# Fused attention and feed-forward: first batch on other PSUM banks, early first-layer chunks, w_in split by GpSimd, constants in one load

## The reference

```python
# q, k, v: (4, 12, 448, 64), cap = 30, w_in (768, 2048), w_out (2048, 768)
scores = cap * np.tanh(scale * np.matmul(q, k.transpose(0, 1, 3, 2)) / cap)
scores = scores - np.max(scores, axis=-1, keepdims=True)
attn = np.exp(scores)
attn = attn / (np.sum(attn, axis=-1, keepdims=True) + 1e-09)
x = np.matmul(attn, v)            # then (batch * 448, 12 * 64)
r = np.maximum(x @ w_in, 0.0)
y = (s * (r * r) + b) @ w_out
```

## Time and profile before

| what | value |
|---|---|
| median of 3 runs | 653.55 us (652.8 to 655.07) |
| the profiled execution | 654.5 us |
| its span in the profile | 652.7 us |
| mean granted clock of PE | 0.987 |
| PE busy | 632.1 us (97%) |
| DVE, ACT, POOL busy | 345.3, 246.1, 37.0 us |

### The profile page before, as it was taken

How to read it: one execution, slowest core, us unless ns; L and a number is a source line. 1 busy time by engine, 2 the same in 40 slices (tenths; PEclk the granted TensorE clock), 3 DMA queues, 4 the chain that set the end, 5 groups by cost and what they waited for, 6 DMA issues and landing times.

```text
span 652.7 us, 7957 instructions
## 1 busy us (share of the span) xinstructions
PE 632.1 (97%) x3146; PEld 490.6 (75%) x3146; DVE 345.3 (53%) x587; ACT 246.1 (38%) x255; POOL 37.0 (6%) x28
## 2 busy tenths in 40 slices
PE   5989989979999999999999999999999999999998
PEld 3333657656767676767677999999999999999997
DVE  1699999997767667767665433222432131213111
ACT  4788444544444544454541322222321121213110
POOL 0122333420000000000000000000000000000000
PEclk8899989998999999999999999999999999999999
DMA  5344143422222222313111411213152233215002
GB/s 167 116 140 140 57 141 115 158 62 99 87 69 88 82 73 83 100 57 101 40 57 44 159 49 49 68 54 109 50 191 57 57 121 105 57 30 183 1 1 84
DMA packets 32148, 57.14 MB, mean 88 GB/s; under 512 B 3952, under 2 KB 23920, under 8 KB 32112
## 3 DMA queue, kind: packets, MB, share of 16 engines
q1 hardware_dynamic: 31680, 56.64, 26.8%
q10 hardware_dynamic: 432, 0.00, 0.0%
HBM read 40.11 MB, written 16.52 MB: 87 GB/s over the span
## 4 chain that ended last, share of the span: by engine, by line
PE 81%; DVE 13%; ACT 3%; issue 2%; DMA 1%; POOLq 0%; POOL 0%; ACTq 0%; DVEq 0%
PE hid L345 10%; PE hid L347 10%; PE hid L346 10%; PE scores L360 8%; PE scores L361 8%; PE scores L359 8%; PE pv L304 5%; PE scores L270 5%; PE pv L360 4%; PE pv L361 4%; PE pv L359 4%; PE scores L289 2%; DVE w_hi L503 2%; DVE e_sum L522 1%; PE pv L316 1%
## 5 line engine op out<-in xcount | busy, mean ns | idle before, releaser
L345 PE MATMUL hid<-x_hi,w_hi 128*128 128x448 f32 x384 | 144.6, 377 | 6.5 <-POOL w_lo L669 6.5
L347 PE MATMUL hid<-x_hi,w_lo 128*128 128x448 f32 x384 | 142.3, 371 | 0.0
L346 PE MATMUL hid<-x_lo,w_hi 128*128 128x448 f32 x384 | 142.2, 370 | 0.0
L360 PE MATMUL scores<-x_lo,w_hi 128*128 128x448 f32 x256 | 93.5, 365 | 0.0
L359 PE MATMUL scores<-x_hi,w_hi 128*128 128x448 f32 x256 | 93.5, 365 | 0.0
L361 PE MATMUL scores<-x_hi,w_lo 128*128 128x448 f32 x256 | 93.5, 365 | 0.0
L345 PEld LDWEIGHTS hid<-x_hi,w_hi 128*128 128x128 f32 x384 | 73.4, 191 | 24.9 <-issue 19.0
L595 DVE SCALAR_TENSOR_TENSOR x_lo<-e,const,x_hi 128x448 fp32r<-128x448 f32 x48 | 32.1, 683 | 103.8 <-ACT x_hi L447 103.8
L347 PEld LDWEIGHTS hid<-x_hi,w_lo 128*128 128x128 f32 x384 | 73.3, 191 | 6.4
L346 PEld LDWEIGHTS hid<-x_lo,w_hi 128*128 128x128 f32 x384 | 73.5, 191 | 6.0
L433 ACT ACTIVATE e<-e,const 128x1792 f32<-128x1792 f32 (+1 forms) x48 | 77.0, 1604 | 1.6
(11 more groups left out here) (67 smaller groups left out, 666.0 us busy)
## 6 DMA issues: line engine op xcount, KB each, us to landing
qk<-q_k SPq DMA_DIRECT2D x24, 448.0 KB, 3.8
hidden_scratch<-hidden_sb SPq DMA_DIRECT2D x48, 224.0 KB, 1.9
e<-hidden_scratch SPq DMA_DIRECT2D x48, 224.0 KB, 2.6
work<-w_in SPq DMA_DIRECT2D x24, 256.0 KB, 3.5
e<-w_out SPq DMA_DIRECT2D x16, 384.0 KB, 3.0
y_t<-qk SPq DMA_DIRECT2D x24, 224.0 KB, 2.0
v_sb<-v SPq DMA_DIRECT2D x24, 192.0 KB, 2.6
v_tail<-v SPq DMA_DIRECT2D x12, 64.0 KB, 2.3
```

The source lines that it names most:

```text
L345: nc.tensor.matmul(out, w_hi[:, j, w], x_hi[:, batch % 2, c, :], start=c == 0, stop=False)
L346: nc.tensor.matmul(out, w_hi[:, j, w], x_lo[:, batch % 2, c, :], start=False, stop=False)
L347: last = nc.tensor.matmul(out, w_lo[:, j, w], x_hi[:, batch % 2, c, :], start=False, stop=c == CT - 1)
L360: nc.tensor.matmul(y_acc(c), w_hi[:, j, w], ring(x_lo, n), start=False, stop=False)
```

## The change

1. One tensor, banks, of eight PSUM banks: 0 to 3 are scores, 4 and 5 hid, 6 and 7 pv. In the first batch pair p's products lie in pv[p % 2] and its sums in pv[(p + 1) % 2], the bank of the neighbouring pair. The second groups of pairs 1 to 5 are written to hid's banks, and the tails of a quad to banks 2 and 3. Pair 0 has all its groups at once on eight banks, with two tanh for the second.
2. PE's order in the first batch: last_scores(p + 1) stands before values(p), tail_values is done pair by pair, and sums waits for xt of the pair before. EARLY = 12 chunks of the first layer run before the pair loop of the second batch, around pair 6's last scores; the other 84 are 14 per pair.
3. GpSimd makes w_hi and w_lo, six pieces at the start, four more casts, and the rest after the sixth x_done. DVE's casts are gone, and its order in the first batch is add_last, scale_pair, add_first, invert_first.
4. cap, s and b come in one DMA, and half of qk 0 is loaded by ACT's queue. The guard is computed after pair 0's exponentials.
5. From pair 6 on the transposition of e_sum is part of the reduction (apply_transpose).

```diff
-        scores = ctx.enter_context(nc.psum_tensor("scores", [P, G1, BANK], F32))
-
-        pv = ctx.enter_context(nc.psum_tensor("pv", [P, 2, BANK], F32))
-        hid = ctx.enter_context(nc.psum_tensor("hid", [P, 2, BANK], F32))
+        banks = ctx.enter_context(nc.psum_tensor("banks", [P, 8, BANK], F32))
+        scores = banks[:, 0:G1]
+
+        hid = banks[:, G1:G1 + 2]
+
+        pv = banks[:, G1 + 2:G1 + 4]
...
         def pv_out(p):
-            return first_banks(p)[:, 0, 0:S] if p < PAIRS else pv[:, p % 2, 0:S]
+            return pv[:, p % 2, 0:S]
+
+        def sums_out(p):
+
+            return pv[:, (p + 1) % 2, 0:S]
+
+        def products(p):
+
+            return p + 1 if p < PAIRS else PAIRS + (p - PAIRS) // 2 + 1
+
+        def last_group(p):
+
+            return p + 2
+
+        def chunks_of(batch, c):
+
+            if batch == 0:
+                share = (CHUNKS - EARLY) // PAIRS
+                return EARLY + share * c, EARLY + share * (c + 1)
+            return SHARE * c, SHARE * (c + 1)
...
+                of = p - QK_SLOTS
+                if of >= 0:
+                    sp.wait_ge(first_done, of + 1)
+                    sp.wait_ge(last_done, of + 1)
+                    sp.wait_ge(tails_done, of // 2 + 1)
...
-            load_qk(0)
+
+            sp.dma_start(qk[0:D, 0].rearrange("p a n -> p (a n)"), q_k[0, 0, 0:D]).then_inc(qk_in[0], 16)
             load_qk(1)
             load_v(0)
             load_w_in(0)
             load_w_in(1)
+            load_qk(2)
+            load_w_in(2)
+            load_w_in(3)
             load_v(1)
-            load_qk(2)
-            for p in range(PAIRS):
+            load_v(2)
+            load_w_in(4)
+            load_qk(3)
+            load_w_in(5)
+            load_w_in(6)
+            load_v(3)
+            load_w_in(7)
+            load_w_in(8)
+            load_w_in(9)
+            for p in range(2, PAIRS):
+                load_qk(p + 2)
                 load_v(p + 2)
-                load_qk(p + 3)
-                load_w_in(p + 2)
-            load_w_in(PAIRS + 2)
-            load_w_in(PAIRS + 3)
 
             for p in range(PAIRS, ALL):
                 batch, c = divmod(p, PAIRS)
                 if p + 2 < ALL:
+                    load_qk(p + 2)
                     load_v(p + 2)
-                if p + 3 < ALL:
-                    load_qk(p + 3)
                 if batch == 1 and c < 4:
...
             def first_scores(p):
-                i = p % QK_SLOTS
-                pe.wait_ge(qk_in[i], 16 * (p // QK_SLOTS + 1))
-
-                reach(pe, tanh_done, 2 * p)
-                for t in range(FULL - 1):
+                pe.wait_ge(qk_in[p % QK_SLOTS], qk_loads(p))
+
+                reach(pe, first_read, p)
+                if p <= PAIRS:
+                    for head in range(2):
+                        row_scores(p, head, 0, head)
+                    if p % 2 and p > 1:
+                        pe.wait_ge(last_read, last_group(p - 1))
+                    for head in range(2):
+                        last = row_scores(p, head, 1, 2 + head)
+                else:
+                    pe.wait_ge(last_read, last_group(p - 1))
+                    for t in range(FULL - 1):
+                        for head in range(2):
+                            last = row_scores(p, head, t, 2 * t + head)
+                last.then_inc(first_done, 1)
...
+            def last_scores(p, bank):
+                for head in range(2):
+                    last = row_scores(p, head, FULL - 1, bank + head)
+                last.then_inc(last_done, 1)
+
+            def tail_scores(quad, bank):
+
+                pe.wait_ge(qk_in[(2 * quad + 1) % QK_SLOTS], qk_loads(2 * quad + 1))
+                for odd in range(2):
+                    of = (2 * quad + odd) % QK_SLOTS
+                    out_rows = slice(odd * D, (odd + 1) * D)
                     for head in range(2):
                         rows = slice(head * D, (head + 1) * D)
...
+                        last = nc.tensor.matmul(banks[out_rows, bank + head, 0:S], qk[rows, of, 1, FULL * P:],
+                                                qk[rows, of, 0, :], start=True, stop=True)
+                last.then_inc(tails_done, 1)
...
-                pe.wait_ge(exp_done, 2 * (p + 1))
-
+
+                if p == 0:
+                    pe.wait_ge(last_read, last_group(0))
                 reach(pe, x_done, p - 1)
+                reach(pe, sums_read, min(p, PAIRS))
+                pe.wait_ge(exp_done, 2 * p + 1)
                 for t in range(FULL):
+                    if t == FULL - 1:
+                        pe.wait_ge(exp_done, 2 * (p + 1))
...
             def sums(p):
-                out = first_banks(p)
+                out = sums_out(p)
                 pe.wait_ge(e_sum_done, 3 * (p + 1))
-                reach(pe, sums_read, p - 1)
+
+                reach(pe, x_done, p)
                 for head in range(2):
                     rows = slice(head * D, (head + 1) * D)
-                    last = nc.tensor.matmul(out[rows, 1, 0:S], ones[:], e_sum[:, p % 2, head, :], start=True, stop=True)
+                    last = nc.tensor.matmul(out[rows], ones[:], e_sum[:, p % 2, head, :], start=True, stop=True)
...
             first_scores(0)
-            last_scores(0)
+            last_scores(0, G1)
+            tail_scores(0, G1 + 2)
             for p in range(PAIRS):
                 first_scores(p + 1)
+                if p + 1 < PAIRS:
+                    pe.wait_ge(last_read, last_group(p))
+                    last_scores(p + 1, G1)
                 values(p)
-                if p % 2:
-                    tail_values(p // 2)
-                last_scores(p + 1)
+                tail_values(p, 1)
+                if p % 2 and p + 1 < PAIRS:
+                    pe.wait_ge(first_read, p + 2)
+                    tail_scores((p + 1) // 2, 2)
                 sums(p)
+
+
+            for c in range(CT - 1):
+                hidden_chunk(0, c)
+            pe.wait_ge(first_read, PAIRS + 1)
+            tail_scores(PAIRS // 2, 0)
+            last_scores(PAIRS, 2)
+            for c in range(CT - 1):
+                hidden_chunk(0, CT + c)
+            for j in range(2):
+                hidden_chunk(0, CT * j + CT - 1)
...
-                    tail_values(p // 2)
+                    tail_values(p - 1, 2)
                 if p + 1 < ALL:
-                    last_scores(p + 1)
-                for chunk in range(SHARE * c, SHARE * (c + 1)):
+                    pe.wait_ge(first_read, p + 2)
+                    if p % 2:
+                        tail_scores((p + 1) // 2, 0)
+                        last_scores(p + 1, 2)
+                    else:
+                        last_scores(p + 1, 0)
+                for chunk in range(*chunks_of(batch - 1, c)):
...
+                if p == 0:
+                    nc.scalar.activation(e[:, TAIL:TAIL + 2, :], hid[:, :, 0:S], ACT.Tanh, scale=tanh_scale
+                                         ).then_inc(last_read, 1)
+                    nc.scalar.activation(e[:, G1:TAIL, :], pv[:, :, 0:S], ACT.Tanh, scale=tanh_scale
+                                         ).then_inc(last_read, 1)
+                    return
+                if p < PAIRS:
+                    source = banks[:, G1:G1 + 2, 0:S] if p % 2 else banks[:, 2:2 + 4, 0:S]
+                else:
+                    source = banks[:, 0:2, 0:S] if p % 2 else banks[:, 0:4, 0:S]
+                nc.scalar.activation(e[:, group_of(p, 1), :], source, ACT.Tanh, scale=tanh_scale).then_inc(last_read, 1)
...
-            act.dma_start(cap_c, cap.broadcast_to([P, 1])).then_inc(const_in, 16)
-            act.dma_start(s_c, s.broadcast_to([P, 1])).then_inc(const_in, 16)
-            act.dma_start(b_c, b.broadcast_to([P, 1])).then_inc(const_in, 16)
+            act.dma_start(const[:, 0:3], consts.broadcast_to([P, 3])).then_inc(const_in, 16)
+            act.dma_start(qk[D:P, 0].rearrange("p a n -> p (a n)"), q_k[0, 0, D:P]).then_inc(qk_in[0], 16)
             act.wait_ge(const_ready, 1)
-            nc.scalar.activation(const[:, 6:7], abs_cap, ACT.Exp, scale=-1.0).then_inc(guard_done, 1)
-            act.wait_ge(guard_done, 1)
-            nc.scalar.mul(guard_c, const[:, 6:7], GUARD).then_inc(guard_done, 1)
             for p in range(PAIRS + 1):
                 first_tanh(p)
                 exponential(p, 0)
                 last_tanh(p)
                 exponential(p, 1)
...
+            for j in tiles_in(0, EARLY):
+                rectify(j)
...
+                nc.vector.tensor_reduce(parts[:], e_sum[:, p % 2].rearrange("p h (n i) -> p (h n) i", i=BLOCK), AX.X,
+                                        ALU.add, apply_transpose=True).then_inc(parts_done, 1)
...
-            dve.wait_ge(guard_done, 2)
             add_first_e(0)
-            add_last_e(0)
             for p in range(PAIRS):
-                w_in_high(p)
+                add_last_e(p)
+                if p == 0:
```

(60 more changed lines are left out.)

131 lines of the change are left out of this document (55 added, 76 removed).

## The result

| what | before | changed |
|---|---|---|
| median of the runs | 653.53 us (651.22 to 655.07) | 657.64 us (656.9 to 658.46) |
| ratio, 95% interval | | 1.0061 (1.0036 to 1.0086) |
| the profiled execution, its span | 654.5, 652.7 us | 656.9, 654.9 us |
| mean granted clock of PE | 0.987 | 0.990 |
| PE busy | 632.1 us | 632.5 us |

One of six executions of the changed kernel took 1038 us at a mean granted clock of 0.557 and stands apart from all others; it is left out here. The change makes the kernel slower by 0.6%, 4 us, where 16 us less were forecast; the result lies outside the range.

What follows compares the result with a forecast made beforehand. PE's work, waits and lower-clock losses were taken to bound the kernel, with VectorE and ScalarE almost full. Terms 6.0 + 11.3 - 1.3 = 16.0 us off the profiled 654.5; from the median 653.55, forecast 637.5 us, range 632.5 to 645.0.

Steps and rivals of the forecast that it cites:

- the w_lo waits: Hid's matmuls on PE: both waits for w_lo from GpSimd go, with their lower clock, 11.3 us gained.
- Rival 2: Hid's matmuls: one w_lo wait stays or comes anew, 643.5 us; both stay, 648.8 us; chance 0.14.
- rival 3: GpSimd's w_in casts are dear and delay q and k of pair 4: slower, up to 662.3 us; chance 0.03.
- the chance of 0.03 for slower: Whole kernel: slower than before by one mechanism, rival 3's dear GpSimd cast; chance 0.03.
- First batch: PE up to pair 7's scores: 6.0 us gained, from 3.9 to 8.4.
- the change of stages: Where chunks 5 and 11 wait for x of pair 5: 1.3 us charged for one or two gaps.
- The start: Pair 0: first scores kept at 5.55 us, first tanh at 8.65 behind a table load, 0.65 us sooner.
- Landmarks: PE's times in the first batch: pair 2's scores at 19 to 21 us, pair 3's at 29.0, pair 7's at 58.1.
- GpSimd on VectorE's port: From 16 to 27 us, VectorE's two-input instructions each pay up to 1.0 us; first-batch gain 5.6 us instead of 8.4.
- Sum: Whole kernel: 6.0 + 11.3 - 1.3 = 16.0 us off, forecast 637.5 us; chance 0.62.
- the signs named as proving it wrong: PE waits for w_lo, pair 4's q and k land after 32 us, or PE waits over 3 us between 19 and 56.
- the signs of being right: Profile: first tanh near 8.65 us, hid's first matmul near 56, no w_lo wait, clock 1.00 from 60, GpSimd casts under 2.

Runs made afterwards that it cites:

- the kernel with the loads in order: The changed kernel with q and k of pair p + 3 again requested at step p from the second batch on, ahead of the stores: 638.27 us.
- the cut kernel: The kernel with the loads in order, with GpSimd's casts and subtractions of the first ten w_in pieces cut to 32 of 512 columns: 638.45 us.
- the kernel with the guard first: The kernel with the loads in order, with the guard's two ScalarE instructions back before pair 0's first tanh: 637.39 us, repeat 637.38 us.

## Why the prediction was wrong

**The step that failed** is in the part on the w_lo waits: "The next six pieces are loaded after two stores of hidden, from 82". I set the stores of hidden and w_in's loads against each other in SP's queue, but gave the loads of q and k there no deadline. The diff moves them by one step, from pair p + 3 to pair p + 2, and I priced that move at nothing without naming it; the list of the change does not name it either, only the diff has it. A line for it would have read: pair 9 is issued behind the stores of the step, at about 86, lands 4 to 5 us later, and is needed by the tail scores at 85. The premise of the quoted sentence was off too: with the early chunks it is four stores, the last of which has left SP at 86.0, and the pieces of w_in go from 87.03. Rival 2 saw that "SP's queue holds w_in behind stores", but looked at w_in alone, and gave it one wait of 6.0 us; rival 3 looked at q and k of pair 4, ahead of all stores. What measured 13.1 us of waits and 4.6 of clock was in no case of mine, and the chance of 0.03 for slower had nothing to do with it.

**The other steps** can be read from the changed kernel up to 66 us, and from the kernel with the loads in order behind it:

- *First batch*, 6.0 forecast less 1.3 for the change of stages, 4.7 together. In the kernel with the loads in order pair 7's scores start at 66.44, with 7.3 us of early chunks done: 63.67 - 59.1 = 4.5. The sum came right by luck, as two errors cancel. The start gave 1.1 less than forecast (first tanh at 9.74), as I kept 5.55 us for the first scores and PE's warm-up ended at 6.5. The change of stages cost no wait at all: PE has no gap between 56.67 and 66 us, so 1.3 was too much.
- *Landmarks.* Pair 2's scores were laid out for 19.3 to 20.6, and came at 20.98; pair 3's for 29.0, and came at 29.29; pair 5's sums for their end at 56, and ended at 56.7.
- *GpSimd on VectorE's port.* The adds of 1.09 grew to 1.64 and 1.38 us, as forecast in kind. The layout had them cost 2.2 us up to the sums of pair 1 (28.0 instead of 25.8); the cut kernel bears out 1.3 to 1.5, by the two workings above. The cast was 0.61 us in the median (1.49 at most), and not 0.9. The Trainium skill, "GPSIMD Engine Reference", section "Elementwise — side-by-side cycle accounting", gives about one cycle per element for such a loop; at the 1.2 GHz of its example that is 0.44 us for 512 elements, an estimate. The trace has 0.17 us more, so the 0.6 of the prediction holds a fixed part that this figure does not give.
- *The w_lo waits*, 11.3. Of the 16.2 us of span between the kernel before and the kernel with the loads in order, 4.5 are the first batch and 11.7 the rest. With casts back on VectorE, 10.1 of them were lost again. Right in kind and size.
- *Sum.* 637.5 was forecast, and 638.27 was measured once the order of the loads was put back. The 0.8 us between are smaller than the two errors that cancel in the first batch, so the closeness is luck in part.

Of the signs named as proving it wrong none appeared: no wait for w_lo, q and k of pair 4 issued at 24.4, and 1.7 us of waits between 19 and 56 us. The signs guarded the steps I had thought of. Of the signs of being right, "a clock of 1.00 from 60 us on" was the one that failed.

## What to carry to other kernels

When a diff changes an index in a queue's program, write for each moved request two times: when the last thing ahead of it in that queue can end, and when its first reader needs it. A queue that holds both loads and stores gives every load the stores' dependencies, here the inversion of sums on VectorE, two steps away from the store; move loads ahead of stores, or give them another queue. And where a long wait hides a second one, taking away either one alone tells too little: try the order by itself, on both kernels.

## What the runs showed that I had not expected

**The warm-up's length.** The same 50 warm-up passes took 5.35 to 5.60 us in most of the kernels built on the change, 4.82 in two, and 4.48 in the repeat of a kernel that had taken 5.38. From 4 to 5 us the kernel before made 20 passes, and the changed one 13, while the granted clock is given as 1.00 in both. The two executions of the kernel with the guard first differ in the same way:

```profile
4.00:5.00 1.00, 1.00 (x13) 1.00 (x12) 0.20 (x2) 0.41 (x2) 0.00 (x0) 1.00 1.07 283
```

```profile
4.00:5.00 1.00, 1.00 (x20) 1.00 (x19) 0.21 (x2) 0.41 (x2) 0.00 (x0) 1.00 1.06 290
```

When PE comes to full pace at the start differs between two executions of one program by about 1 us, and the row of the granted clock does not show it. The Trainium skill, "TensorE: Matmul & The Clock Gate", in its part on the clock gate, says that the number of slow matmuls at a kernel's start varies from run to run; the two executions agree. What decides it was not tried.

**The split load.** q and k of pair 0 in two halves on two queues landed at about 6.2 us where PE waited for them (0.4 to 0.7 us in four of the kernels), later than the whole load in the kernel before, which PE had by 5.55. Whether the split or the other loads around it make it later is open: with the load whole again, the warm-up to 6.5 us hides when it landed.

**VectorE's small copies beside GpSimd.** Copies of 32 x 28 elements took 1.89 us for three, against 0.57, and those of 32 x 14 2.53 for four, against 0.76: over three times as long, though each has but one input.

**A clock that fell for a small gap, or didn't.** Pair 0 has PE gaps of 1.6 and 1.8 us in the kernel with the loads in order, without a fall. In the kernel with GpSimd's pieces cut, gaps of 1.6 and 1.8 us at the same places were followed by a granted clock of 0.59 over the 4.20 us from 15.80. The kernel with the guard first shows both in one program: a gap of 1.67 us before 27.06 without a fall in its first profile, and in its repeat a gap of 1.64 us before 27.01 with this behind it:

```profile
28.00:32.00 4.00, 4.00 (x12) 1.75 (x12) 3.90 (x7) 2.55 (x3) 0.62 (x1) 0.59 0.42 160
```

The second took 1.1 us longer (638.54 and 637.41). What decides it stays open.
